# Batched attention and two MLP stages on one core: earlier first tokens, and another table of weight units

## The reference

```python
q_s = softmax(q, axis=-1);  k_s = softmax(k, axis=2)       # k over the tokens
x = einsum('bhsd,bhde->bhse', q_s, einsum('bhsd,bhse->bhde', k_s, v))
x = x.transpose(0, 2, 1, 3).reshape(B, S, 512)
u = x + (relu(x^T @ w_tok1) @ w_tok2)^T                    # mixing over tokens, 576 -> 256 -> 576
y = u + relu(u @ w_ch1) @ w_ch2                            # 512 -> 1536 -> 512
out = y + relu(layernorm(y, g_ln) @ w2_ch1) @ w2_ch2       # 512 -> 2048 -> 512
```

## Time and profile before

| what | value |
|---|---|
| median of three timed runs | 1591.9 us |
| profiled execution: its time, its span | 1593.26 us, 1591.5 us |
| TensorE busy | 1488.4 us (94%), 7584 matmuls |
| VectorE, ScalarE, GpSimd busy | 69%, 44%, 19% |
| DMA, mean over the span | 270 GB/s |
| mean granted TensorE clock | 0.981 of full speed |

### The profile page before, as it was taken

How to read it: one execution, slowest core, us unless ns; L and a number is a source line. 1 busy time by engine, 2 the same in 40 slices (tenths; PEclk the granted TensorE clock), 3 DMA queues, 4 the chain that set the end, 5 groups by cost and what they waited for, 6 DMA issues and landing times.

```text
span 1591.5 us, 19837 instructions
## 1 busy us (share of the span) xinstructions
PE 1488.4 (94%) x7584; PEld 1332.6 (84%) x7584; DVE 1091.0 (69%) x1165; ACT 698.0 (44%) x844; POOL 308.3 (19%) x315
## 2 busy tenths in 40 slices
PE   6999977889989989999989999999999999999998
PEld 5998876778878867878978888888888888889998
DVE  7988866497379378388588578568757865873276
ACT  5656644353353354254353454245335434532342
POOL 5687775431213122220000000000000000000000
PEclk9999988999999999999999999999999999999999
DMA  8889885998879988988757767876876687667766
GB/s 242 255 296 288 285 286 188 391 332 324 314 281 339 341 309 301 344 326 304 264 206 269 248 233 240 266 253 204 281 239 244 225 268 247 222 218 244 258 211 202
DMA packets 150334, 429.28 MB, mean 270 GB/s; under 512 B 14240, under 2 KB 43488, under 8 KB 150240
## 3 DMA queue, kind: packets, MB, share of 16 engines
q1 hardware_dynamic: 132768, 361.94, 66.5%
q0 software_dynamic: 17472, 66.07, 11.6%
HBM read 348.26 MB, written 79.69 MB: 269 GB/s over the span
## 4 chain that ended last, share of the span: by engine, by line
PE 70%; DVE 12%; DMA 10%; issue 4%; ACT 2%; POOL 1%; SPq 1%; DVEq 0%; ACTq 0%; POOLq 0%
PE ps L1132 23%; PE ps L1134 22%; PE ps L1133 22%; DMA w_ring<-w_scratch_B 7%; DVE x_lo L833 2%; DVE o_lo L981 2%; DMA qt<-q 2%; DVE q_sum L760 1%; POOL q_lo L461 1%; PE ps L1156 1%; PE ps L1167 1%; DVE h L967 1%; DVE qt L777 1%; DVE h L951 1%; DVE q_den L768 1%
## 5 line engine op out<-in xcount | busy, mean ns | idle before, releaser
L1132 PE MATMUL ps<-o_hi,w_ring 128*128 128x462 f32 (+1 forms) x980 | 371.0, 379 | 34.9 <-DVE o_lo L981 22.9
L1132 PE MATMUL ps<-x_hi,w_ring 128*128 128x462 f32 (+1 forms) x980 | 368.7, 376 | 22.4 <-DMA w_ring<-w_scratch_B 11.7
L1133 PE MATMUL ps<-o_lo,w_ring 128*128 128x462 f32 (+1 forms) x980 | 367.4, 375 | 0.0
L1134 PE MATMUL ps<-x_hi,w_ring 128*128 128x462 f32 (+1 forms) x980 | 367.3, 375 | 0.0
L1134 PE MATMUL ps<-o_hi,w_ring 128*128 128x462 f32 (+1 forms) x980 | 367.0, 375 | 0.0
L1133 PE MATMUL ps<-x_lo,w_ring 128*128 128x462 f32 (+1 forms) x980 | 366.8, 374 | 0.0
L674 ACT CAST o_hi<-h 128x924 fp32r<-128x924 f32 (+1 forms) x210 | 202.0, 963 | 264.5 <-PE ps L1134 225.5
L981 DVE TENSOR_TENSOR o_lo<-h,o_hi 128x924 fp32r<-128x924 f32 (+1 forms) x210 | 247.0, 1179 | 65.3 <-ACT o_hi L674 65.2
L1132 PEld LDWEIGHTS ps<-o_hi,w_ring 128*128 128x128 f32 x980 | 186.7, 191 | 70.1 <-issue 33.5
L1132 PEld LDWEIGHTS ps<-x_hi,w_ring 128*128 128x128 f32 x980 | 186.2, 190 | 51.4 <-issue 23.2
L951 DVE TENSOR_TENSOR h<-ps,h 128x924 f32<-128x924 f32 (+1 forms) x90 | 100.5, 1117 | 174.5 <-PE ps L1134 174.2
(11 more groups left out here) (140 smaller groups left out, 1842.7 us busy)
## 6 DMA issues: line engine op xcount, KB each, us to landing
w_ring<-w_scratch_C SPq DMA_DIRECT2D x280, 512.0 KB, 3.8
w_ring<-w_scratch_B SPq DMA_DIRECT2D x210, 512.0 KB, 5.5
w_scratch_C<-w_out POOLq DMA_DIRECT2D x8, 1792.0 KB, 10.9
w_scratch_C<-last_pair POOLq DMA_DIRECT2D x8, 1792.0 KB, 11.6
w_scratch_B<-w_out POOLq DMA_DIRECT2D x6, 1792.0 KB, 9.4
w_scratch_B<-last_pair POOLq DMA_DIRECT2D x6, 1792.0 KB, 9.7
kt<-kT SPq DMA_DIRECT2D x32, 288.0 KB, 6.2
u_scratch<-u_out SPq DMA_DIRECT2D x32, 288.0 KB, 4.9
```

Source lines behind the costliest of these rows:

```text
L1132: mm(dst, a_hi, b_hi, start=start, stop=False, skip_group_check=onto)
L1133: mm(dst, a_hi, b_lo, start=False, stop=False, skip_group_check=onto)
L1134: return mm(dst, a_lo, b_hi, start=False, stop=stop, skip_group_check=onto)
```

## The change

It has three parts. SyncE's four loads of the first tokens move from behind step 6 to ahead of step 4, with their wait for the u stores of batches 0 and 1. The table HI_AT changes: units 8 to 13 are at entries 0, 4, 8, 12, 27 and 36, and then five units a position at its local entries 0, 6, 11, 27 and 36 (four in position 3). And ScalarE's cast of unit 7 moves from the middle of step 7 to its end, while the casts x_hi of products 4, 5 and 6 of the first tokens move into the first call, one behind each of its first three products.

```diff
--- before.py
+++ after.py
@@ -63,8 +63,10 @@
 
 
     UNITS_A = NB
-    HI_AT = {1 + 5 * i: UNITS_A + i for i in range(U0["C"] - UNITS_A)}
-    HI_AT.update({22 + 9 * i: U0["C"] + i for i in range(UNITS["C"])})
+    HI_AT = {e: UNITS_A + i for i, e in enumerate((0, 4, 8, 12, 27, 36))}
+    HI_AT.update({(s + 1) * ENTRIES["B"] + e: UNITS_A + 6 + 5 * s + i
+                  for s in range(3) for i, e in enumerate((0, 6, 11, 27, 36))})
+    HI_AT = {e: u for e, u in HI_AT.items() if u < U0["C"] + UNITS["C"]}
 
     def end(c, q):
 
@@ -316,6 +318,16 @@
                     wait_u(sp, i, 2 * c + 1)
                     sp.dma_start(u_v[:, c, bass.ds(i * S, S)], u_out[:, c, :]).then_inc(u_stored, 16)
 
+            def load_x(pos, c):
+
+                if c == 0 and pos >= NSG:
+                    sp.wait_ge(y_stored, 64 * (pos - NSG + 1))
+                if c == 0 and pos > 0:
+                    sp.wait_ge(x_lo_made, 7 * pos)
+                n = 2 * SIZES[pos % NSG]
+                sp.dma_start(xn[:, c * n:(c + 1) * n], tokens(source["BC"[pos // NSG]], pos % NSG)[:, c, :])\
+                  .then_inc(x_in, 16)
+
             load_q(0, ST, first=True)
             sp.dma_start(tok_raw[:, 0:(NT - 1) * DT].rearrange("p (t n) -> p t n", n=DT),
                          w_tok1[0:(NT - 1) * P, :].rearrange("(t p) n -> p t n", p=P)).then_inc(tok1_in, 16)
@@ -328,6 +340,10 @@
                          w_tok2.rearrange("(t p) n -> p t n", p=P)).then_inc(tok2_in, 16)
             sp.dma_start(gcol[:, :], g_ln).then_inc(gcol_in, 16)
             for i in range(NB - 1):
+                if i == NB // 2:
+                    sp.wait_ge(u_stored, 16 * NC * 2)
+                    for c in range(NC):
+                        load_x(0, c)
                 step(i, 2 if i < NB - 2 else 1)
 
             def load_entry(n):
@@ -343,16 +359,6 @@
                 sp.dma_start(w_ring[:, n % RW, :, :, :].rearrange("p k s f -> p k (s f)").bitcast(fp32),
                              ws_dram[c.stage][local]).then_inc(w_in[n % RW], 16)
 
-            def load_x(pos, c):
-
-                if c == 0 and pos >= NSG:
-                    sp.wait_ge(y_stored, 64 * (pos - NSG + 1))
-                if c == 0 and pos > 0:
-                    sp.wait_ge(x_lo_made, 7 * pos)
-                n = 2 * SIZES[pos % NSG]
-                sp.dma_start(xn[:, c * n:(c + 1) * n], tokens(source["BC"[pos // NSG]], pos % NSG)[:, c, :])\
-                  .then_inc(x_in, 16)
-
             def load_res(pos, c):
 
                 if c == 0 and pos > 0:
@@ -370,9 +376,6 @@
                 sp.dma_start(target[c.stage][:, 2 * i:2 * i + 2, t:t + c.n], quarter(res, c.n, i, half))\
                   .then_inc(y_stored if c.stage == "B" else out_stored, 16)
 
-            sp.wait_ge(u_stored, 16 * NC * 2)
-            for c in range(NC):
-                load_x(0, c)
             for n in range(RW):
                 load_entry(n)
             step(NB - 1, 0)
@@ -625,7 +628,6 @@
                     if later == 0 and c == 0:
                         hi_x(0, 2)
                     if later == 0 and c == 1:
-                        hi_unit(i)
                         hi_x(0, 3)
                 if later:
                     hi_q(i + 1, ST[3:])
@@ -693,14 +695,15 @@
                     nc.scalar.activation(ln[:, 3, 0:2 * n], ln[:, 0, 0:2 * n], ACT.Abs_reciprocal_sqrt)\
                       .then_inc(root_made, 1)
 
-            for p in (4, 5, 6):
-                hi_x(0, p)
+            hi_unit(NB - 1)
             for c in CALLS:
                 if c.j >= 0:
                     last = c.j == G1S[c.stage] - 1
                     for p in range(7):
                         if p in (0, 1, 2, 6):
                             take(c, p)
+                        if c.index == 0 and p < 3:
+                            hi_x(0, 4 + p)
                         if p == 4:
                             relu(c, 4)
                         if p == 5:
```

## The result

| | before | after |
|---|---|---|
| timed runs, median (range) | 1592.0 us (1586.4 to 1592.3, 4 runs) | 1572.9 us (1564.2 to 1579.1, 4 runs) |
| profiled execution, its span | 1593.3, 1591.5 us | 1570.0, 1568.2 us |
| granted clock, mean | 0.981 | 0.990 |

The ratio after to before is 0.9884 with a 95% interval of 0.9837 to 0.9930: the change makes the kernel about 18 us faster (11 to 26). The forecast was 1575. In the code of after, the lines of VectorE and TensorE stand 3 lower than before (L1132 is now L1135).

The account below looks back on a forecast made before the run. TensorE, busy 94% of the span, was taken as the bound: a chain of matmuls with gaps. The terms -10.1 + 5.0 - 4 - 9 = -18 took 1593.3 us to 1575, range 1562 to 1590 (the forecast case's own 1570 to 1582).

Parts of the forecast that it names:

- Part a: Last batch of the first stage: it no longer waits for tokens, -10.1 us (-10.6 to -8).
- entry 1 starts as late as before: Start of position 0: the moved casts leave entry 1 behind VectorE's u copy of chunk 2, no earlier.
- Part b: Middle of the first stage: token loads stand ahead of batch 5's in SyncE's queue, +5.0 us (0 to +6).
- nothing covers the added bytes: Batch 5's loads: 1.89 MB more delay the last q chunk and are not made up later, 5.0 us at 382 GB/s.
- 34 us against 29: First stage: sign that one step takes 34 us where its neighbours take 29.
- Part c: Position 0, entries 0 to 41: earlier units win 7.05 us and lose 3.2, -4 us (-7 to +21).
- ScalarE's take would be what entry 11 waits for last: Position 0: ScalarE, held up at unit 10, frees entry 11's bank near 305.7 instead of 302.5, 3.2 us.
- Part d: Positions 1 to 3: o_lo waits -12, clock -4, new transfer waits +7, together -9 us.
- I am wrong if they pass 30: Whole kernel: sign that the prediction is wrong if w_ring waits pass 30 us in all.
- position 0 stalls ScalarE: Rival in position 0: slow loads for units 9 to 11 hold ScalarE, +21 us there, 1601 in all; chance 0.12.
- the tokens move for nothing: Rival: token loads cost 0 in the middle and the bursts of units return only 2, 1565 us; chance 0.18.
- transfers take the gain back: Rival: position 0 wins 0 and positions 1 to 3 return 14 us, 1586 us in all; chance 0.20.

Follow-up runs that it names:

- 4: Kernel before with only the unit table of positions 1 to 3 changed (position 0's unit at entry 40 moves to 42): 1573.9 us, ratio 0.9903.
- 2: Kernel before with only the first tokens' loads moved ahead of step 4, table and casts as before: 1586.6 us, ratio 0.9983.
- 11: Kernel before with only the order of ScalarE's casts between the stages changed: 1591.8 us, ratio 1.0003.
- 5: Changed kernel with units 8 to 11 of position 0 back at entries 1, 6, 11 and 16: 1572.4 us, ratio 0.9874.
- 1: Changed kernel with the first tokens loaded late again, behind step 6; table and casts stay changed: 1575.9 us, ratio 0.9916.
- Experiment 8: Changed kernel with the four token loads in the same middle step but behind batch 4's k, q and v: 1572.6 us, ratio 0.9870.
- 3: Changed kernel with the token loads in the last batch but one, behind its v: 1564.1 us, ratio 0.9831.
- 10: Changed kernel with two of four token loads left in the middle, the other two in the last batch but one behind v: 1568.3 us, ratio 0.9857.
- 7: Changed kernel with tokens loaded behind v of the last batch but one, position 0's units at 1, 6, 11, 16, 22, 31: 1570.5 us, ratio 0.9846.
- 6: Changed kernel with units 8 to 11 of position 0 at entries 2, 6, 10 and 14: 1566.7 us, ratio 0.9823.
- 9: Changed kernel with tokens loaded behind v of the last batch but one and units 8 to 11 at 2, 6, 10, 14: 1564.1 us, ratio 0.9825.

## Why the prediction was right, step by step

The sum was right: -18 predicted, -19 by the medians. By the experiments it is made up like this: table in positions 1 to 3 -15.4 (4), tokens -2.7 (2), casts 0 (11), units 8 to 11 of position 0 0 (5). These add to -18.1, where 0.9884 of 1590 is -18.4; with intervals of 2.4 us and more on each, so close a fit is chance, and units 12 and 13 were not tried by themselves. The prediction had -9, -5.1, 0 and -4. It named mechanisms that the traces show, but gave 6.4 us too little to the table in positions 1 to 3 and 6.4 too much to tokens and position 0. That these cancel is luck.

**Part a held.** -10.1 predicted, -10.9 in the trace; the tokens alone give 9.1 (42.6 to 33.5 in 2), their removal costs 8.3 (1). The rest is the order of the casts. The wait of entry 1 (4.78 us, 5.23 before) ends 0.09 us behind VectorE's last u copy in both traces, as the prediction said. But the step "entry 1 starts as late as before" was wrong: 2.85 us earlier in 11. It had no effect on the time that can be seen: in the profile of 11 position 0 took it back, which I had not argued.

**Part b: right path, size too large.** +5.0 predicted. In the four profiles with all loads ahead of batch 5's the step takes 31.6 to 33.2 us (mean 32.3), in the eight with none 28.4 to 28.8 (mean 28.7): +3.6. The path was the one named: the last q chunk lands 17.1 us after the batch's first product in those four and 13.6 in the eight, 3.5 later. The term of 5.0 (1.89 MB at 382 GB/s) fits the front of the queue, where the first q chunk lands 5.0 us later (7.02 against 2.05). The mis-sized piece is "nothing covers the added bytes": 1.5 us were made up between the first chunk and the last, in a stretch that the engines had filled to 1.02 at 317 GB/s and in which they moved 352 when more was asked of them. That the higher rate made it up is argued. The forecast "34 us against 29" was 32.0. The stall of VectorE and TensorE in front was not foreseen.
Of the rule in the Trainium skill (page "DMA: Bandwidth & Descriptors", section "Queues, rings and completion order") that a DMA engine takes the descriptors of one queue in ring order, the trace of after agrees. The four token loads landed at 140.3, 141.5, 142.6 and 143.8 us, k's first chunk at 144.5 and q's at 145.1, one behind the other as they were issued, though all six had been issued by 139.1. Had the bytes been shared out evenly, I worked out 2.5 for the delay, and 5.0 if all stood ahead; the first chunk shows 5.0. Experiment 8 says nothing on this: it issues the token loads from 151.2, when the last q chunk had landed (150.2).

**Part c: right number in one profile, not found in the time.** -4 predicted, -4.0 seen in the one profile. Its local effects were there: entry 5 is late (3.1, predicted 2.5), entry 11 too (5.6, predicted 3.2), the waits at 21 and 23 went, and 5 brings the one at 23 back (3.34). That ScalarE's take would be what entry 11 waits for last was 0.6 us off: its load landed behind it. But 1 against 4 hardly leaves room for 4 us in the whole time, and the profiles of the ten kernels with the new table in positions 1 to 3 say the same:

| units 8 to 11 at | kernels | position 0, us | positions 0 to 3, us (mean) |
|---|---|---|---|
| 0, 4, 8, 12 | after, 1, 3, 8, 10 | 125.9 to 127.0 | 475.2 to 484.4 (477.7) |
| 1, 6, 11, 16 | 4, 5, 7 | 127.8 to 129.6 | 473.2 to 480.1 (476.3) |
| 2, 6, 10, 14 | 6, 9 | 121.3 and 126.0 | 475.0 and 477.3 (476.2) |

Position 0 itself is shorter with the early units, the four positions together are not. The step that failed is the one that counts a position as won once its waits are gone: what position 0 wins is not found again at the end of position 3. With the old table in all positions (before, 2, 11) the four take 493.2, 488.1 and 498.7, so the new table in 1 to 3 stands out by some 16 us, as in experiment 4. Position 0 runs at a DMA share of 0.93 as a whole:

```profile
260.00:385.90 125.90, 111.33 (x492) 95.15 (x492) 81.52 (x75) 53.51 (x53) 42.15 (x50) 0.96 0.93 350
385.90:504.10 118.20, 110.13 (x504) 95.22 (x504) 77.43 (x70) 51.25 (x51) 33.69 (x35) 0.99 0.90 331
504.10:619.90 115.80, 109.82 (x504) 95.20 (x504) 75.11 (x71) 51.17 (x51) 32.35 (x35) 0.99 0.93 341
619.90:736.40 116.50, 109.27 (x505) 95.86 (x506) 73.94 (x68) 49.54 (x50) 15.68 (x20) 0.99 0.91 325
```

**Part d held in kind, and was too small.** -9 predicted, -12.8 in the trace of after, -15.4 by experiment 4. The waits for o_lo gave 14.6 where I had 12: the 1 us a position that I left for GpSimd's sums was not needed. TensorE's busy time over positions 1 to 3 went from 333.5 to 329.3 us at the higher clock, 4.2, predicted 4. I had 7 us of new waits for w_ring. By the view's names they stayed at 12 (12.3 and 12.0), but with entries 42, 84 and 126 they are 20.2; before, with one wait of 2.4 (415.35) that a landing at 415.26 ended, they were 14.7. So 5.5 us came, where I had 7. (The largest is at the start of position 1: its load was issued at 376.86 and took 12.9 us to land, with the DMA engines at 1.01 from 360 to 390.) So the mis-sized terms are o_lo and, in experiment 4, the clock as well: there TensorE's busy time fell to 325.0 us, 4.3 below after. The unnamed waits are 4.3 us there, not 8.8, with 1.6 more for w_ring and 1.3 for h; together this is the difference between 12.8 and 18.7. Over the whole span the w_ring waits are 19.2 us by the view and 32.4 with the four that it puts elsewhere (27.0 before, with two), so "I am wrong if they pass 30" was a sign that the view alone could not answer.

**Rivals.** That position 0 stalls ScalarE: it idled 7.63 us before unit 8 and 5.65 before unit 10, but 1.13 before unit 9 and not before unit 11. That the tokens move for nothing: refuted by the step of 32.3 us in four profiles against 28.7 in eight. That transfers take the gain back: in positions 1 to 3 5.5 us came back and not 14; position 0's 4 us are not found in the time.

**What stays open.** Profiles of kernels with the same table in positions 1 to 3 differ there by up to 13 us (344.6 in 4, 358.0 in 8), with one profile each; so whether 6 beats after by its own mechanism, and whether 3 and 6 add, is not settled. Nor is what makes up the 1.5 us in the step from 4 to 5, or why TensorE is late behind v in 10.

No run was faster than experiments 3, 6 and 9, at 0.982 to 0.983: moving the token loads to the last batch but one is the further step with the clearest ground. Its interval (0.9813 to 0.9849) overlaps only at the edge with those of the two kernels that load in the middle (from 0.9837 and 0.9844), and its trace shows the long step gone.

## What to carry to other kernels

A load that nobody waits for still costs the batch behind it in the queue; put it behind the last batch that loads, not merely behind one batch. When a step grows, look for the point from which the rest always takes the same time (here 15.1 us from the last q chunk): a stall ahead of it, even one of 4 us on an engine in order, may cost nothing. Where a row names no releaser, or one that had long been done, look whether a load landed just before. And where several stages share queues that are nearly full, judge a saving by the sum over all of them, against a version that undoes that edit alone: a difference in one position of one pair of profiles can be right to the tenth and not be found in the time.

## What the runs showed of the hardware that was not expected

At a DMA busy share of 1.0 the rate still had room: 317 GB/s before and 352 after in the same 26 us, at shares of 1.02 and 1.05. A full share is thus no proof that added bytes cost their full time to all that stands behind them: 1.89 MB put off the first q chunk by 5.0 us, but the last one by 3.5 and the step by 3.6. And six loads issued on SyncE's queue between 135.75 and 139.1 us landed one behind the other (140.3 to 145.1).
